# Attention of a fused layer: the second projection ahead of the sums, the last turn of results ahead of the outputs

## What is computed

```python
def phi(x):
    proj = np.einsum('bhsd,md->bhsm', x, omega)
    sq = np.sum(x * x, axis=-1, keepdims=True) / 2.0
    h = proj - sq
    h = h - np.max(h, axis=-1, keepdims=True)
    return np.exp(h) / np.sqrt(m)
q_p, k_p = phi(q_s), phi(k_s)
kv = np.einsum('bhsm,bhsd->bhmd', k_p, v)
z = np.sum(k_p, axis=2)
num = np.einsum('bhsm,bhmd->bhsd', q_p, kv)
den = np.einsum('bhsm,bhm->bhs', q_p, z)[..., None] + 1e-06
attn = num / den
x = _moe_ref(attn reshaped to 2304 x 512)     # dense: x @ w_in, gate, @ w_out
out = _moe2_ref(x)                            # the best of 8 experts for each token
```

## Time and profile before

| | |
|---|---|
| median of the three runs | 819.95 us |
| the profiled execution, its time | 821.36 us |
| the profiled execution, first to last instruction (span) | 819.3 us |
| mean granted TensorE clock | 0.986 |
| PE busy, share of the span | 781.3 us, 95% |
| PEld / DVE / ACT / POOL busy | 714.8 / 355.7 / 309.2 / 332.5 us |

### The profile page before, as it was taken

How to read it: one execution, slowest core, us unless ns; L and a number is a source line. 1 busy time by engine, 2 the same in 40 slices (tenths; PEclk the granted TensorE clock), 3 DMA queues, 4 the chain that set the end, 5 groups by cost and what they waited for, 6 DMA issues and landing times.

```text
span 819.3 us, 15762 instructions
## 1 busy us (share of the span) xinstructions
PE 781.3 (95%) x5526; PEld 714.8 (87%) x5527; DVE 355.7 (43%) x905; ACT 309.2 (38%) x718; POOL 332.5 (41%) x285
## 2 busy tenths in 40 slices
PE   7999989999999999999999999996999999999993
PEld 6777777899899989989989989995999999999993
DVE  4767777511234424434433446652762331333231
ACT  3777676633232232232232233252224424325220
POOL 4877776035222222222222232274026726538411
PEclk9999999999999999999999999997999999999997
DMA  7876773011040020020001001411062632521111
GB/s 265 303 257 226 241 271 142 14 39 52 18 163 1 0 77 0 0 77 0 0 22 55 0 0 39 158 49 55 14 243 55 197 111 97 175 58 29 41 45 31
DMA packets 25444, 74.17 MB, mean 91 GB/s; under 512 B 3120, under 2 KB 3632, under 8 KB 25280
## 3 DMA queue, kind: packets, MB, share of 16 engines
q1 hardware_dynamic: 22144, 63.68, 22.2%
q0 software_dynamic: 3264, 10.03, 4.1%
HBM read 61.11 MB, written 12.58 MB: 90 GB/s over the span
## 4 chain that ended last, share of the span: by engine, by line
PE 75%; issue 8%; POOL 7%; ACT 4%; DVE 3%; DMA 1%; SPq 0%; ACTq 0%; DVEq 0%; POOLq 0%
PE pj L703 21%; PE nm L890 14%; PE pj L1296 8%; PE kv L890 7%; PE kv L1312 6%; PE nm L1312 6%; PE nm L1296 5%; POOL gl L860 2%; POOL sqt L206 2%; POOL sqt L202 2%; PE pj L1325 1%; ACT feat L418 1%; PE pj L256 1%; PE tr L1283 1%; PE kv L274 1%
## 5 line engine op out<-in xcount | busy, mean ns | idle before, releaser
L860 POOL TENSOR_TENSOR gl<-g,gh 128x384 fp32r<-128x384 f32 x96 | 100.1, 1046 | 298.3 <-ACT gh L721 298.3
L716 DVE TENSOR_TENSOR g<-pj,sg 128x384 f32<-128x384 f32 x96 | 53.5, 557 | 223.1 <-ACT sg L711 222.9
L711 ACT ACTIVATE sg<-pj 128x384 f32<-128x384 f32 x96 | 47.2, 492 | 253.5 <-PE pj L703 253.5
L703 PE MATMUL pj<-xh,win_h 128*128 128x384 f32 x384 | 129.5, 337 | 1.2 <-DVE xl L738 1.2
L703 PE MATMUL pj<-xh,win_l 128*128 128x384 f32 x384 | 129.4, 337 | 0.0
L703 PE MATMUL pj<-xl,win_h 128*128 128x384 f32 x384 | 128.9, 336 | 0.0
L703 PEld LDWEIGHTS pj<-xh,win_h 128*128 128x128 f32 x384 | 72.2, 188 | 5.2 <-DVE xl L738 1.5
L703 PEld LDWEIGHTS pj<-xl,win_h 128*128 128x128 f32 x384 | 72.1, 188 | 3.6
L703 PEld LDWEIGHTS pj<-xh,win_l 128*128 128x128 f32 x384 | 72.0, 188 | 0.0
L1296 PE MATMUL pj<-xTh,W 128*128 128x288 f32 x320 | 70.4, 299 | 0.0
L826 DVE SCALAR_TENSOR_TENSOR raw<-tr,xT 128x512 f32<-128x512 f32 x90 | 58.6, 688 | 8.4 <-DVE g L716 7.6
(11 more groups left out here) (245 smaller groups left out, 1736.7 us busy)
## 6 DMA issues: line engine op xcount, KB each, us to landing
wraw<-in_moe_w SPq DMA_DIRECT2D x7, 2048.0 KB, 10.5
ve<-in_v_z SPq DMA_DIRECT2D x16, 585.0 KB, 3.8
qk<-in_qk_n SPq DMA_DIRECT2D x16, 576.0 KB, 5.0
qkT<-in_qk_t SPq DMA_DIRECT2D x15, 576.0 KB, 5.5
y_rows<-ys SPq DMA_DIRECT2D x18, 256.0 KB, 2.4
stage<-in_moe_w_in SPq DMA_DIRECT2D x8, 512.0 KB, 6.4
y_early<-ys SPq DMA_DIRECT2D x12, 256.0 KB, 2.7
stage<-in_moe_w_out SPq DMA_DIRECT2D x4, 512.0 KB, 6.3
```

The costliest lines, as they stand in the source:

```text
L703: mm = eng.matmul(ph[f % 3][:, 0:BT], w[f // F1A][:, c, f % F1A, :], x[:, c, :], start=(c == 0 and w is win_h and x is xh), stop=(c == DC ...
L711: eng.activation(sg[f % 2][:, :], ph[f % 3][:, 0:BT], ACT.Sigmoid, scale=1.702).then_inc(a_sg, 1)
L716: eng.tensor_tensor(g32[f % 2][:, :], ph[f % 3][:, 0:BT], sg[f % 2][:, :], ALU.mult).then_inc(v_g, 1)
L860: eng.tensor_tensor(gl[f % 3][:, :], g32[f % 2][:, :], gh[f % 3][:, :].bitcast(F32), ALU.subtract).then_inc(g_gl, 1)
```

## The change

On PE `project(x, 1)` moves from behind `sums` to ahead of it in every step, and in even steps `turn_x(2)` moves from between the two outputs to ahead of both. On ACT, in even steps, `copy_x(1)` and `copy_qf(2)` come ahead of `exps_b(x, 1)`, and `copy_x(2)` ahead of `exps_a(x, 1)`. No instruction is added or removed, and DVE, POOL and SP keep their programs.

```diff
@@ tensor: step
             project(*x, 0)
+            project(*x, 1)
             sums(i, n, a)
-            project(*x, 1)
             turn_qf(i, n, a, 0, before)
             project(*x, 2)
@@
             turn_qf(i, n, a, 2, before)
-            output(i, n, a, 0)
             if before:
                 turn_x(n - 1, 2, i)
+            output(i, n, a, 0)
             output(i, n, a, 1)
@@ scalar: step
             copy_qf(i, n, a, 1, before)
+            if before:
+                copy_x(n - 1, 1)
+                copy_qf(i, n, a, 2, before)
             exps_b(*x, 1)
             if before:
-                copy_x(n - 1, 1)
-            copy_qf(i, n, a, 2, before)
+                copy_x(n - 1, 2)
+            else:
+                copy_qf(i, n, a, 2, before)
             exps_a(*x, 1)
-            if before:
-                copy_x(n - 1, 2)
```

## The result

The changed kernel takes 821.15 us (median of 12 runs, 820.73 to 822.06), the kernel before 819.87 us (median of 12 runs). The ratio of the undisturbed runs is 1.0024, with a 95% interval of 1.0016 to 1.0032: the change costs 0.24%, or 2.0 us of 819.9 (1.3 to 2.6). The two medians differ by less, 1.28 us. By the 2% that the prediction took as what can be told, it is no change. One run of the kernel before, at 1043.7 us, was disturbed and is left out of the ratio. The forecast was 2.65 us slower, 822.6 us.

The account below looks back on a forecast made before the run. The prediction took a loop through DVE, PE's turn of results, ACT and POOL's squares as the bound. 5 x 0.45 = 2.25 us plus 0.4 us gave 2.65 us slower, 822.6 us; range 818 to 826 us.

Parts of the forecast that it names:

- Item 1: ACT, even steps: copy_x(1) waits for PE's second turn, so exps_b of group 2 starts 0.45 us later (0.14 to 0.57).
- Item 2: PE, end of even steps: turn_x(2) waits for copy_x(1), 0.38 us later; lies beside ACT's delay, the larger counts.
- with the same work behind it: PE, end of even steps: after turn_x(2) starts 0.38 us later, PE's remaining work was taken as unchanged.
- Item 3: PE, every step: project(x, 1) ahead of the sums leaves PE's work the same; gain counted as 0.
- The thin cover of 0.07 us: PE, odd steps: exps_b of group 2 ends at 79.22, PE arrives at 79.29; if gone, waits up to some 0.3 us.
- Items 4 and 5: Sums end 0.87 us later, absorbed by ACT's idle time; SP's next qk load still lands 2.5 us early; both cost 0.
- Steps 12 to 14: Steps 12 and 14, without address work between wait and copy: PE's delay about 0.2 us each, 0.4 us together.
- The small gain through DVE's wait for `project(x, 1)`: Rival, odd steps: top(x, 1)'s 0.39 us wait saved in six steps, 2.3 us, 817.6 us; chance 0.14 with its strong form.
- PE's gaps: Strong form of the faster rival: 1.39 us of gaps close in seven pairs, 9.7 us, 810.2 us; together chance 0.14.
- The late sums: Rival: copy_kv holds ACT past the turns, steps 1 to 14 lose up to 0.87 us, 12.2 us, 832.1 us; chance 0.10.
- the late loads: Rival: a qk load 3.5 us slower holds POOL up 1.0 us, 6 us in six pairs, 826 us; chance 0.04.

Follow-up runs that it names:

- `pool_late`: POOL's low parts moved one step later, behind the next squares, against the kernel before: 817.53 us, ratio 0.9990.
- `tail_only`: ACT's new order and turn_x(2) ahead of both outputs, without moving project(x, 1), against the kernel before: 821.96 us, ratio 1.0035; on top of `pool_late` 819.03 us.
- `p1_only`: Only project(x, 1) moved ahead of the sums on PE, against the kernel before: 818.88 us, ratio 0.9993.
- the probes: `pool_late` with project(x, 1) ahead of the sums, plus one unused 128-row matmul behind the two projections (817.58 us) or between them (820.29 us).

## Why the prediction was right, and where it was not

**The bound.** The prediction held that a pair closes on itself from `norms` through the turn of results, ACT and POOL's squares, and not through PE, the fullest engine. The chain of the changed kernel shows the same loop, `pool_late` opens it, and `tail_only` on top of `pool_late` costs 0.09 us a pair where it costs 0.3 us with the loop closed. What the prediction did not see is how close behind the loop PE's row stands: 0.24 us a pair. The `norms` are 18.48 us apart, at the lower end of the 18.5 to 18.7 us that it named. The range of 818 to 826 us holds the kernel before as well, so that the time alone says little for the mechanism; the single changes do.

**Item 1, ACT's order.** The mechanism and its place were right, down to the term: `exps_b` of group 2 starts 2.29 us behind the start of `copy_x(1)` (77.22 - 74.93), as worked out. The time from PE's turn to that copy was mis-sized: I took 0.33 us from the waits ahead of the first copy, and it is 74.93 - (74.25 + 0.55) = 0.13 us. So the term is 0.12 + 0.13 = 0.25 us and not 0.45 us. The pair became 0.29 us longer; the other 0.04 us I did not follow. Five pairs cost 1.68 us, not 2.25 us. This is about half of the error.

**Item 2, PE's turn behind the copy.** Right in kind: `turn_x(2)` waits 0.23 us and `output(0)` does not wait. But "with the same work behind it" was wrong. The third turn and the two outputs take 78.04 - 76.21 = 1.83 us before and 77.15 - 75.47 = 1.68 us after: 0.15 us of PE's row fall away in a pair with the outputs side by side. Their matmuls have 64 columns (128*64 in the rows), those of the turn 128; whether that is the reason was not tried.

**Item 3, `project(x, 1)` ahead.** The thin cover of 0.07 us was gone, and PE waits 0.20 us for `exps_b`; as foreseen that costs nothing while POOL sets the pair. The gain was put at 0, with the reason that only the order of two blocks is swapped and PE's work is the same. That step was wrong: PE's work is 0.35 us shorter, since two changes between 64 and 128 rows fall away. It shows in step 1, which POOL does not set (-0.35 us), and it is hidden in the pairs; in odd steps of the loop nearly all of it is lost again to the wait for `exps_b` (1.86 against 1.54 us up to the sums in `p1_only`). The Trainium skill, TensorEngine Tiling (Array Packing), Key Properties, states that a change of the tiling mode drains TensorE; the probes agree, with 0.39 us for two changes; that it is a drain they do not show. I had not weighed that rule, and it speaks for this change.

**Items 4 and 5, the late sums and SP's queue.** Both held. ACT waits 0.89 us for the sums in odd steps and still 0.52 us behind that for the turn. No squares in the looped steps waited for a `qk` load in the changed kernel. With POOL's squares early they do: `pool_late` has nine such waits between 37 and 140 us, 16.9 us in all, and its chain over the same time does not go through POOL.

**The sum.** 2.65 us by the prediction, 1.53 us by the trace, 2.0 us (1.3 to 2.6) by the runs. It took the lag of item 1 too large (0.57 us of the 1.12 us of difference) and left out what PE saves in step 1 (0.35 us). Steps 12 to 14 cost 0.20 us and not 0.4 us. The dense layer starts at 154.18 us and not at 156.9: the loss was 1.12 us smaller, and the start of this execution 1.55 us shorter.

**The rivals.** The small gain through DVE's wait for `project(x, 1)` did not come, for the reason given: 18.23 us a pair in `p1_only`. By the rule that one should work on the most occupied engine, PE's gaps should have been worth 9.7 us; on the kernel as it was, `project(x, 1)` ahead brought 0.03 us a pair and 0.77 us in all by the trace, which the runs do not tell from nothing (0.9983 to 1.0003). Once POOL is out of the loop, work on PE does pay: the same move then brings 4.1 us. The Trainium skill, Perfetto Trace Analysis, Identifying the Most-Contended Engine, which the prediction names there, judges TensorE by its weight loads and its useful work, not by its matmul time. By its weight loads PE has 13.94 us of the pair and POOL 14.09 us, so that the rule did not point to PE as clearly as the prediction had it. The late sums and the late loads did not come through.

## What to carry to other kernels

Follow the loop that a pair of steps closes on itself before moving work on the fullest engine: here the row of the fullest engine became 0.35 us shorter in a step and 0.03 us a pair came through, because of a loop through an engine that is busy for 78% of the time; with that loop opened it was 0.53 us a pair. On an engine that works in order, don't put a copy that has to wait for another engine ahead of work that is ready, where a loop runs through that engine; one such swap cost 0.27% of the whole kernel. Where matmuls of fewer rows can stand together, put them together, and count the changes between the two kinds in TensorE's row as work.

## What was not expected of the hardware

A change of TensorE between matmuls of 64 rows in pairs and matmuls of 128 rows costs about 0.2 us at 2.4 GHz (0.39 us for two in the probes, at a granted clock of 1.00). It is no row of its own and shows only in the distance of starts: in step 1, from the first projection to the third, 28.17 - 23.75 = 4.42 us before and 26.27 - 22.20 = 4.07 us after, for the same matmuls. And the time from the end of a turn on PE, as the profile has it, to ACT's copy is not one number: it was 0.21 to 0.45 us for the first copy of an even step in the loop with weights, 0.13 us for the second, and 0.02 us for the first in step 12. What sets it apart was not tried.
